# Attention rebuilt on four heads at a time: scores by 64x64 tiles in TensorE's row halves, wider copies, two MLP steps per unit

## What is computed

```
B, H, S, D = 4, 8, 576, 64;  window = 64
scores = q @ k.T / sqrt(D), masked to 0 <= rel < window
attn = softmax(scores);  x = attn @ v            # x: (2304, 512)
x = (sigmoid(x @ w_gate) * (x @ w_val)) @ w_out  # 512 -> 1536 -> 512
out = ((x @ w_a) * (x @ w_b)) @ w_out2           # 512 -> 1536 -> 512
```

## Time and profile before

| | |
|---|---|
| median of 3 runs | 998.49 us (996.11 to 999.04) |
| profiled execution, its own time | 1000.73 us |
| its span, first to last instruction | 998.9 us |
| mean granted TensorE clock | 0.991 |
| PE busy | 967.7 us (97% of the span) |
| DVE / ACT / POOL busy | 683.9 / 524.4 / 194.7 us |

### The profile page before, as it was taken

The page is one execution under the profiler, slowest core; times in us unless marked ns, Lnnn a source line. Parts: engine busy times, 40 slices in busy tenths (PEclk is TensorE's granted clock), DMA queues, the critical chain, the costliest instruction groups (busy, mean ns, idle before and its releaser), DMA issues.

```text
span 998.9 us, 16028 instructions
## 1 busy us (share of the span) xinstructions
PE 967.7 (97%) x5700; PEld 887.2 (89%) x5700; DVE 683.9 (68%) x1496; ACT 524.4 (53%) x1014; POOL 194.7 (19%) x276
## 2 busy tenths in 40 slices
PE   5899999999999999999989999999999999999998
PEld 5698887888878888888889899999999999999998
DVE  5777778777686776766656667685756757664756
ACT  3678768676686766644434434434344435253233
POOL 4023343322233222433335300000000000010000
PEclk8899999999999999999999999999999999999999
DMA  8747785767747676564558759676688667677662
GB/s 201 185 132 227 223 231 170 204 191 222 223 146 214 192 221 196 162 235 167 178 178 299 266 213 355 225 261 256 245 312 281 237 246 276 222 291 269 235 245 114
DMA packets 150544, 223.36 MB, mean 224 GB/s; under 512 B 84929, under 2 KB 104385, under 8 KB 148161
## 3 DMA queue, kind: packets, MB, share of 16 engines
q1 hardware_dynamic: 135104, 171.99, 52.2%
q0 software_dynamic: 15360, 50.34, 15.6%
HBM read 179.83 MB, written 42.47 MB: 223 GB/s over the span
## 4 chain that ended last, share of the span: by engine, by line
PE 86%; ACT 3%; DVE 3%; DMA 3%; issue 2%; POOL 1%; SPq 1%; DVEq 0%; POOLq 0%; ACTq 0%
PE ps L615 13%; PE ps L729 13%; PE ps L731 13%; PE ps L730 13%; PE ps L617 13%; PE ps L616 13%; PE ps L578 3%; PE ps L607 2%; PE ps L588 2%; DMA w_raw<-in_moe_w_out 1%; DMA k_nat<-in_k 1%; ACT p_out L868 1%; PE ps L564 1%; DMA out<-ost 1%; ACT probs L814 1%
## 5 line engine op out<-in xcount | busy, mean ns | idle before, releaser
L615 PE MATMUL ps<-x_hi,gv_hi 128*128 128x512 f32 (+1 forms) x480 | 185.6, 387 | 5.0 <-DVE hid L1111 4.1
L617 PE MATMUL ps<-x_hi,gv_lo 128*128 128x512 f32 (+1 forms) x480 | 178.2, 371 | 0.0
L616 PE MATMUL ps<-x_lo,gv_hi 128*128 128x512 f32 (+1 forms) x480 | 177.6, 370 | 0.0
L729 PE MATMUL ps<-xc,wc 128*128 128x384 f32 x504 | 171.3, 340 | 0.0
L731 PE MATMUL ps<-xc,wc 128*128 128x384 f32 x504 | 170.3, 338 | 0.0
L730 PE MATMUL ps<-xc,wc 128*128 128x384 f32 x504 | 170.2, 338 | 0.0
L238 POOL DMA_DIRECT2D w_raw<-in_moe_w_gate x60 | 46.1, 769 | 375.6 <-DVE wo_lo L1102 362.7
L1198 DVE TENSOR_TENSOR tt<-ps,tt 128x384 f32<-128x384 f32 x108 | 59.3, 556 | 86.2 <-PE ps L731 85.9
L615 PEld LDWEIGHTS ps<-x_hi,gv_hi 128*128 128x128 f32 x480 | 91.2, 190 | 15.7 <-issue 6.1
L617 PEld LDWEIGHTS ps<-x_hi,gv_lo 128*128 128x128 f32 x480 | 90.8, 189 | 11.9
L616 PEld LDWEIGHTS ps<-x_lo,gv_hi 128*128 128x128 f32 x480 | 91.2, 190 | 9.5
(11 more groups left out here) (104 smaller groups left out, 1799.0 us busy)
## 6 DMA issues: line engine op xcount, KB each, us to landing
wc<-wprep SPq DMA_DIRECT2D x54, 1024.0 KB, 6.8
wc<-wprep SPq DMA_DIRECT2D x54, 768.0 KB, 5.7
wprep<-p_out SPq DMA_DIRECT2D x18, 1792.0 KB, 7.9
w_raw<-in_moe_w_gate POOLq DMA_DIRECT2D x60, 256.0 KB, 3.3
w_raw<-in_moe_w_val POOLq DMA_DIRECT2D x60, 256.0 KB, 3.6
w_raw<-in_moe_w_out POOLq DMA_DIRECT2D x60, 256.0 KB, 4.7
v_nat<-in_v SPq DMA_DIRECT2D x64, 128.0 KB, 3.8
k_nat<-in_k SPq DMA_DIRECT2D x40, 128.0 KB, 4.0
```

The lines of the kernel that those rows point to most:

```text
L615: pe.matmul(dst, w_h, m_h, start=first, stop=False)
L616: pe.matmul(dst, w_h, m_l, start=False, stop=False)
L617: return pe.matmul(dst, w_l, m_h, start=False, stop=last)
L729: pe.matmul(dst, w_h, m_h, start=k in (0, 1, 3) and t == 0, stop=False, skip_group_check=True)
```

## The change

A unit becomes a *double*: four heads (two pairs p, each of two heads r) and the same 192 queries; there are 24. `q_diag` is gone. q and k of a pair stand transposed with one head in partitions 0 to 63 and the other in 64 to 127, and `score` makes 12 matmuls, each with 64 rows (the half of the head r), 64 stationary columns (the pair p chooses the half of the PSUM partitions) and 128 moving columns; the two heads r go to two PSUM banks. `fill` is 8 transposes, `turn` 6, `mix` 12 matmuls. `unfill` is one DVE operation of 384 columns, `copy_k` one ACT copy of 512, `turned_copy` one of 768 out of two banks, `mix_hi` and `mix_lo` one of 384 each, and `normalise` in the chunks is 3 operations for all four heads (768 columns). The mask, maximum and exponentials are as many as before.

A double starts at every even step of chunks 0 to 2 and at steps 0 and 2 of chunk 3. In its step `fill` stands between the two `up`s and `score` behind the second (in step 0 of a chunk: before the first and between them); `turn` is in the next, odd step before `down`, and `mix` at the start of the step after that. The first 4 doubles run alone. v has two buffers in place of three. Preparations stand at even steps from 2 to 46 without multiples of 8, all 18 before chunk 4. In chunk 4 the first inputs of the second MLP (`x_hi_of`, `x_sum`, `x_lo_of`) are made from step 4 on in place of step 7, and their load is issued at step 2 in place of 4.

```diff
-PREP_EVERY, PREP_FROM = 3, 3
+PREP_STEPS = [s for s in range(2, 4 * STEPS, 2) if s % 8 != 0]
...
+        def doubles_before(c):
+            return min(FIRST_DOUBLES + c * STEPS // 2, DOUBLES)
...
+                self.fill_bank = n % 2 * 2 if early else ATT_BANK
+                self.score_bank = GATE_BANK if early else ATT_BANK
+                self.probs = probs_b if early and n % 2 else probs_a
+                self.at = (n // 2 * UQ + RING_AT) % RING
...
+        def double_of(c, f):
+            if f % 2 or c > 3 or c == 3 and f > 2:
                 return None
-            if isinstance(c, int):
-                u = units_before(c) + unit_at(c, f) + ahead
-                return Unit(u) if u < UNITS else None
-            return Unit(units_before(1) + f + ahead, c - 1)
+            return Double(doubles_before(c) + f // 2)
...
+            if i >= V_BUFS:
+                eng.wait_ge(mixed, i - V_BUFS + 1)
...
+                if s % 2 == 0:
+                    i = s // 2 + FIRST_DOUBLES
+                    if i < DOUBLES:
+                        load_v(sp, i)
+                    if i + 2 < DOUBLES:
+                        load_qk(sp, i + 2)
...
+            def score(d):
+                pe.wait_ge(unfilled, d.n + 1)
+                pe.wait_ge(k_copied, d.n + 1)
+                if d.early and d.n >= 1:
+                    pe.wait_ge(maxed, 2 * d.n)
                 for i in range(UB):
-                    mm = pe.matmul(bank(u.score_bank, i * P, (i + 1) * P), q_diag[:, u.slot, i, :],
-                                   k_t[:, u.slot, i * QB:i * QB + P], start=True, stop=True)
+                    for p in range(2):
+                        for r in range(2):
+                            dims = slice(r * HD, (r + 1) * HD)
+                            mm = pe.matmul(ps[p * QB:(p + 1) * QB, d.score_bank + r, i * P:(i + 1) * P],
+                                           q_t[dims, d.slot, p, i * QB:(i + 1) * QB],
+                                           k_t[dims, d.slot, p, i * QB:i * QB + P], start=True, stop=True)
                 mm.then_inc(scored, 1)
...
+                to_turn = to_mix = None
                 for f in range(STEPS):
                     s = c * STEPS + f
-                    unit = unit_of(c, f)
-                    if before:
-                        mix(before)
-                    if unit:
-                        score(unit)
+                    d = double_of(c, f)
+                    if to_mix:
+                        mix(to_mix)
+                        to_mix = None
                     if f == 0:
-                        pe.wait_ge(mixed_lo, units_before(c))
+                        pe.wait_ge(mixed_lo, doubles_before(c))
+                        if d:
+                            fill(d)
                     up(s, f, 0, x_off, w)
-                    if unit and unit_of(c, f, 1):
-                        fill(unit_of(c, f, 1))
+                    if d:
+                        score(d) if f == 0 else fill(d)
                     up(s, f, 1, x_off, w)
-                    if unit:
-                        turn(unit)
+                    if d and f > 0:
+                        score(d)
+                    if to_turn:
+                        turn(to_turn)
+                        to_mix = to_turn
+                    to_turn = d
...
+                        copy_k(d)
+                    if f + 1 < STEPS or c < CHUNKS - 1:
                         split_gv(c, f + 1)
-                    if unit:
-                        exps(unit)
                     split_wo(s, f)
                     open_gate(s, w)
+                    if d:
+                        if f > 0:
+                            copy_k(d)
+                        exps(d, 0)
+                        exps(d, 1)
                     if prep_at(s - 1) is not None:
                         weights_hi(prep_at(s - 1))
-                    if unit:
-                        turned_copy(unit)
-                    if isinstance(c, int) and c == CHUNKS - 1:
-                        if f == 7:
+                    if to_turn:
+                        turned_copy(to_turn)
+                        to_mix = to_turn
+                    to_turn = d
...
+                    if d and f == 0:
+                        unfill(d)
+                    if f + 1 < STEPS or c < CHUNKS - 1:
                         split_gv(c, f + 1)
-                    if unit and unit_of(c, f, 1):
-                        unfill(unit_of(c, f, 1))
-                    if unit:
-                        normalise(unit)
+                    if d and f > 0:
+                        unfill(d)
+                    if to_turn:
+                        normalise(to_turn, 0, 2)
+                        to_mix = to_turn
                     split_wo(s, f)
+                    if d and f == 0:
+                        mask_and_max(d, 0)
+                        mask_and_max(d, 1)
                     if prep_at(s - 1) is not None:
                         weights_lo(prep_at(s - 1))
                     hidden(s, f, w)
-                    if isinstance(c, int) and c == CHUNKS - 1:
-                        if f == 7:
+                    if d and f > 0:
+                        mask_and_max(d, 0)
+                        mask_and_max(d, 1)
+                    to_turn = d
...
+            mask_and_max(first[0], 0)
+            mask_and_max(first[0], 1)
+            unfill(first[2])
+            normalise(first[0], 0, 1)
+            normalise(first[0], 1, 1)
+            mask_and_max(first[1], 0)
+            mask_and_max(first[1], 1)
+            unfill(first[3])
+            mix_lo(first[0])
+            normalise(first[1], 0, 1)
+            normalise(first[1], 1, 1)```

DVE in a step of chunk 0 or later, before. `gap` and the two `L1051` rows are `mask_and_max`, then come `split_gv`, `unfill` of the next unit, `normalise`, `split_wo` and `hidden`.

```order
L1047 MEMSET gap 1x1 [waits scored]
L1051 ISA probs,neg_max<-ps,mask 128x128
L1051 ISA neg_max 128x1
...
L1088 TENSOR_TENSOR gv_lo<-w_raw,gv_hi 128x1024 [waits gv_hi_ready]
L1071 TENSOR_SCALAR q_diag<-ps 64x3x64 [waits filled]
...
L1075 COPY k_t<-ps 128x256
L1057 TENSOR_SCALAR row_inv<-row_sum 128x3 [waits exped]
L1060 RECIPROCAL row_inv<-row_inv 128x3 [waits summed]
L1063 TENSOR_TENSOR probs<-probs,row_inv 128x384 [waits inverted]
L1102 TENSOR_TENSOR wo_lo<-w_raw,wo_hi 128x512 [waits wo_hi_ready]
```

More of the change, by code:

```diff
@@ L246, in prep_at @@
         def prep_at(s):
[L248 to L249 removed]
+            return PREP_STEPS.index(s) if s in PREP_STEPS else None
         def prep_block(t, i, j):
@@ L514, in _ @@
             load_v(sp, 1)
-            for i in range(2, FIRST_UNITS // 2):
-                load_qk(sp, i + 1)
-                load_v(sp, i)
-            load_v(sp, FIRST_UNITS // 2)
-            load(FIRST_UNITS // 2 + 1)
+            load_qk(sp, 3)
+            load_v(sp, 2)
+            load_qk(sp, 4)
+            load_v(sp, 3)
+            load_qk(sp, 5)
             load_weights(0)
@@ new lines, in turn @@
+            def turn(d):
+                pe.wait_ge(normed, 2 * d.n + 2)
+                if d.early and d.n >= 1:
+                    pe.wait_ge(turned_out, d.n)
+                    pe.wait_ge(mixed_lo, d.n)
+                for r in range(2):
+                    for i in range(UB):
+                        mm = pe.transpose(bank(ATT_BANK + r, i * P, (i + 1) * P), d.probs[:, r, i * P:(i + 1) * P],
+                                          ident[:, :])
+                mm.then_inc(turned, 1)
@@ new lines, in mix @@
+            def mix(d):
+                pe.wait_ge(v_in[d.v_buf], V_IN * d.v_loads)
+                pe.wait_ge(turned_out, d.n + 1)
+                for p in range(2):
+                    for i in range(UB):
+                        for r in range(2):
+                            head = slice((2 * p + r) * HD, (2 * p + r + 1) * HD)
+                            mm = pe.matmul(ps[r * HD:(r + 1) * HD, ATT_BANK, p * UQ + i * QB:p * UQ + (i + 1) * QB],
+                                           v_nat[:, d.v_buf, i, head],
+                                           probs_t[:, r, i * P + p * QB:i * P + (p + 1) * QB],
+                                           start=True, stop=True)
```

428 lines of the change are left out of this document (193 added, 235 removed).

## The result

The changed kernel takes 1013.58 us (median of 4 runs, 1012.42 to 1014.47) against 998.76 us for the kernel before on the same chip: a ratio of 1.0153, 95% interval 1.0132 to 1.0175. It is slower. The forecast was 992.6 us, faster, and its range ended at 1004. The profiled execution, itself 1014.16 us long, has a span of 1012.38 us from its first to its last instruction.

What follows compares the result with a forecast made beforehand. PE was taken to bound nearly every stage. Stage terms 7.5 - 2 - 5.4 - 1 - 5 = -5.9 us, taken from the median 998.49, gave 992.6 us, with an 8-in-10 range of 983 to 1004.

Steps and rivals of the forecast that it cites:

- What bounds the kernel, who waits: PE busy nearly throughout; odd step's turn just in time at 512 columns, 1.4 us late per chunk 0 double.
- The PE terms of a double: Fill 0.78, turn 0.67, mix 0.98, score 0.9: 3.33 us per double against 4.15, if nobody waits.
- The rival of the score in line: Row halves don't overlap: score 2.9 to 3.1 us, 2.0 more for 14 doubles, 1026 us in all; chance 0.12.
- the floor: Score's matmuls run four at a time, six slots of 0.13 us, some 0.9 us with the stops at either end.
- POOL's sums: Sums falling on `hidden` in even steps: 0 to 0.9 us per double, 0.5 taken for 9 doubles in chunks 1 to 3.
- The start: Before chunk 0: third double's fill ahead of scored work; first gate product at 47.5 to 48 us, +7.5 us.
- Chunk 4: Three preparations move ahead of it, 2.3 us left for the load of x: -5 us.
- the signs of being wrong that I named: Score over 1.4 us, PE waiting over 1 us for chunk 1's turn, or start ending under 43 or over 51.
- Rival 4: Chain later than worked out, by table load or gate wait: 1 us more on 20 doubles, 1005 us; chance 0.12.

Runs made afterwards that it cites:

- e3_sums_behind: Changed kernel with one wait more: GpSimd starts a preparation's sums only when that step's low part of the hidden values is written; 993.0 us, ratio 0.9951.
- e8_one_tile: Changed kernel with normalisation ahead of the weights' low part, reordered start, sums behind hidden values, and the score one 64x64 tile at a time; 1000.07 us.
- e4_rows_apart: Changed kernel with the score's 24 matmuls reordered, all of the lower row half, then all of the upper; 1013.62 us.
- e6_no_last: Changed kernel with normalisation ahead of the weights' low part, reordered start, sums behind hidden values, no preparation in a chunk's last but one step; 980.65 us.
- e10_late: Kernel of e3_sums_behind with two unused reductions on DVE ahead of the normalisation in chunk 0's odd steps; 1017.55 us, ratio 1.019.
- e7_before_placed: Kernel before with only the changed kernel's steps for the preparations; 999.66 us, ratio 1.0009.
- e1_norm_first: Changed kernel with VectorE normalising, in odd steps, ahead of the low part of the next gate and value weights; 997.57 us, ratio 0.999.

## Why the prediction was wrong

**What bounds the kernel, who waits.** Right. PE bounds every stage, and the turn of the odd step is what waits, for `probs_a`. Without the sums it waits only at 384 columns, 1.5 us at most and 7.5 in six waits (e3_sums_behind), against 1.4 forecast for each; at 512 columns the chain is just in time, as forecast.

**The PE terms of a double.** Right. Mix 0.92 against 0.98, score 0.89 against 0.9, and a pair of steps without a wait 19.92 against 2 x 8.29 + 3.33 = 19.91. The rival of the score in line would have been smaller than I had it, too: one tile at a time costs 1.69 us, 0.8 more, not 2. The reason that I gave for the score was weaker than its result. I read from `mix` that column halves overlap, since its 12 records of 64 columns took 0.57 us where a full tile's price would make 0.78. But a lone 64x64 tile takes 0.07 us for a record of 128 columns (e8_one_tile); at that price the 12 records would need some 0.4 us in line (an estimate; a tile of 128 rows and 64 columns was not run alone). So that row does not show overlap by itself, and that the floor came true was in part luck. What shows it is the score itself: 0.89 us against 1.15 (e4_rows_apart) and 1.69 (e8_one_tile).

**POOL's sums: the step that failed.** I took 0.5 us for each of 9 doubles in chunks 1 to 3 and 1.2 in all for chunk 0, with 0.9 per double as the upper bound, from one `h_hi`: 5.7 us in all. The one wait of e3_sums_behind shows that they cost 20.6. Three things were off. The size: an ordinary pair with sums lost 1.07 us, over my upper bound, by `h_hi` and `h_lo` together; and in two steps of chunk 0 `h_lo` went from 0.56 to 2.88 us, two and a half times my bound. The number: 11 doubles of chunks 1 to 3 waited, not 9. And the ends of chunks 1 and 2, where `h_lo` took 2.98 us, the turn waited 1.98, and in chunk 1 the last step fell from 16.34 to 14.07 us once the sums were moved (from this step's gate start to the next one's). By stages, the two steps of chunk 0 make 8.9 us and chunks 1 to 3 11.3.

So 14.9 of the 21.0 us that I missed by are the sums. The stages of e3_sums_behind, set against the forecast without its 5.7 us, hold the rest: chunks 0 to 3 are 5.6 us longer, of which 3.5 are four waits for `h_lo` at the ends of chunks that I did not have, the start is 1.0 longer, chunk 4 and the second MLP 3.0 shorter. The remaining 2.5 us are the distances of the profiled executions from their medians: 2.2 above in the kernel before, 0.25 below in e3_sums_behind.

The Trainium skill states this cause: "SBUF — State Buffer", section "Who interferes with whom", has a VectorE instruction with two SBUF inputs contend with a GpSimd instruction that reads SBUF, and one with at most one SBUF input not, unless it runs in one of VectorE's two-port modes. The trace agrees for `h_lo` (2.88 us) and for the mask (0.28 us, no change). `h_hi` reads one SBUF operand and is slowed as well, 0.43 to 1.29 us; whether it runs in a two-port mode no run here shows. The same section has whoever comes first hold the shared ports for its whole instruction, with the other fully blocked. The rows of e6_no_last fit that roughly: `gv_lo`, 1.22 us alone, begins at 156.10 and ends 1.1 us after the end of the second sum at 156.77, and the third sum, 0.74 alone, ends 0.6 us after `gv_lo`, as if the two took turns. Who comes first is less clear: `h_lo` began at 90.71, 0.34 us ahead of the first sum, and was the one held, until about the end of the third; but POOL was then issuing a DMA (from 90.48), and its sums follow on that without a pause.

**The price of a wait: a term that I had at nothing.** I priced a late turn at its own length. From 9.55 us (e3_sums_behind) to 14.54 the odd step grew by 5.0 for a wait that grew by 2.3; the other 2.7 are 12 down products at 0.32 in place of 0.17 us, with turn and mix at half clock. A wait of 1.5 us had no such tail. e10_late shows it with the sums out of the way. Two such steps explain 8.9 us of chunk 0 (14.54 and 13.42 against 9.55 twice).

**The start.** +9.9 against +7.5. The reason was right (fill of the third double, whose keys come at 17.1, ahead of scored work), its size 2.4 short, or 1.0 by e3_sums_behind, whose start is the same program and took 49.02. The first gate product came at 50.4, inside the 43 to 51 that I had named.

**Chunk 4.** -7.3 against -5. I had left 2.3 us for the load of x; the chunk has no idle time at all. e7_before_placed shows that the gain is the placement's, and that the placement also has a price at each end of a chunk (about 1 to 2 us), which I had not seen: the preparation's low part stands ahead of the last hidden values.

**The rivals.** Of the signs of being wrong that I named, one came: the turn waited 1.98 us at the end of chunk 1. Rival 4, a later chain, was the nearest in kind: it had 1 us on each of 20 doubles and the time at 1005. It named a table load or a gate wait as the cause, and had no clock in it. Above all, "the chain has no reserve" stood in the text, and a chain without reserve turns every unknown on it into time, so I should have given it more than 0.12.

What stays open: why the second MLP, the same program, varies between 410.4 and 412.5 us, why the start of e8_one_tile is longer by more than its scores, and why some waits near 2 us drop the clock and others do not (below).

## What to carry to other kernels

When work is regrouped into fewer, larger pieces, the engine total may fall just as computed and the chain between two pieces may still decide; list everything on it and ask of each operation what other engine's work the new order puts beside it. Work of GpSimd that reads SBUF should be made to wait, if need be by a semaphore, until the VectorE operations on the critical chain that it was seen to slow, here the rounded copy and the remainder of the hidden values, are over. And a wait of TensorE of some 3 us or more has to be priced with the slow products behind it.

## What the runs showed of the hardware

- Fp32 matmuls in 64x64 tiles, 24 of 128 columns each: 0.89 us with all four tiles in turn, 1.15 with a pair that differs in columns, 1.69 with the same tile six times running. The Trainium skill, "TensorE: Matmul & The Clock Gate", part 3, has 3.07 times for four small tiles in row groups; here the score as a whole gains 1.9 times over one tile at a time, as even a lone tile takes 0.07 us a record, about half of the 0.13 of a full one.
- One `tensor_tensor` of VectorE, the same shape in the same place: 0.56 us alone, 2.88 us under GpSimd's sums. A cast of 512 columns: 0.43 alone, 1.29 under them.
- Waits of TensorE of 3.8 us were followed by 3 to 6 us at 0.50 of the clock (0.50 from 100 to 106 us in the one case, 0.50 from 124 to 126 and 1.00 from 127 in the other), waits of 1.5 us in e3_sums_behind by none. Between them it differs: 1.90 and 2.24 us in e1_norm_first had slow products behind them, 1.98 in the changed kernel and 2.40 in e7_before_placed did not.
